# First group of a delta-rule attention: 16x16 lane inverses joined on TensorE, and its later pieces moved among its steps

## The reference, cut to what matters

```python
k_n = k / (np.linalg.norm(k, axis=-1, keepdims=True) + 1e-06)
for t in range(S):
    kt, vt, bt = (k_n[:, :, t], v[:, :, t], beta[:, :, t, None])
    y[:, :, t] = np.einsum('bhd,bhde->bhe', q[:, :, t], state)
    v_old = np.einsum('bhde,bhd->bhe', state, kt)
    state = state + bt[:, :, :, None] * np.einsum('bhd,bhe->bhde', kt, vt - v_old)
```

## Time and profile before

| | |
|---|---|
| median of 3 runs | 909.62 us (909.47 to 911.56) |
| profiled execution, its own time | 913.28 us |
| its span | 911.5 us |
| PE busy (92%) | 837.3 us |
| DVE busy | 477.4 us |
| ACT busy | 301.5 us |
| POOL busy | 199.2 us |
| DMA queue q1, 32802 packets | 63.85 MB |
| DMA queue q8, kind "instruction", 69 packets | 1.13 MB |

### The profile page before, as it was taken

How to read it: one execution, slowest core, us unless ns; L and a number is a source line. 1 busy time by engine, 2 the same in 40 slices (tenths; PEclk the granted TensorE clock), 3 DMA queues, 4 the chain that set the end, 5 groups by cost and what they waited for, 6 DMA issues and landing times.

```text
span 911.5 us, 24639 instructions
## 1 busy us (share of the span) xinstructions
PE 837.3 (92%) x10634; PEld 811.5 (89%) x10634; DVE 477.4 (52%) x1092; ACT 301.5 (33%) x654; POOL 199.2 (22%) x167
## 2 busy tenths in 40 slices
PE   6378889899986799999999999999999999999998
PEld 6268888898885799999999999999889999899898
DVE  5999987979465574424442543433542432432421
ACT  4147374656532212211111211123441331331422
POOL 3123122031200530800270010000132222132231
PEclk9657787987978799999999999999999999999999
DMA  9600506134145121022000201201510010000001
GB/s 362 164 37 23 202 30 196 37 106 140 64 160 165 53 63 59 18 70 69 17 9 9 69 17 49 78 16 64 194 53 27 26 52 26 26 0 26 27 1 53
DMA packets 32889, 65.13 MB, mean 71 GB/s; under 512 B 3673, under 2 KB 25506, under 8 KB 32802
## 3 DMA queue, kind: packets, MB, share of 16 engines
q1 hardware_dynamic: 32802, 63.85, 20.8%
HBM read 46.86 MB, written 14.16 MB: 67 GB/s over the span
## 4 chain that ended last, share of the span: by engine, by line
PE 60%; issue 21%; DVE 11%; ACT 4%; POOL 2%; DMA 1%; SPq 1%; POOLq 0%; ACTq 0%; DVEq 0%
PE m_ps_h L1090 12%; PE g_ps_v L1601 11%; PE m_ps_d L1090 10%; PE ps_ga L404 4%; PE g_ps_y L1601 3%; PE ps_y L495 3%; PE ps_y L490 3%; DVE t_lane L584 2%; DVE prod L580 2%; PE ps_u L473 2%; PE ps_r L455 2%; POOL g_vn_lo L1498 2%; PE g_ps_u L1601 2%; PE ps_s L508 2%; ACT tt L327 2%
## 5 line engine op out<-in xcount | busy, mean ns | idle before, releaser
L1090 PE MATMUL m_ps_h<-m_unt_hi,m_w_hi 128*128 128x256 f32 x432 | 122.3, 283 | 2.8 <-DVE m_unt_lo L1280 2.1
L1090 PE MATMUL m_ps_h<-m_unt_lo,m_w_hi 128*128 128x256 f32 x432 | 121.4, 281 | 0.0
L1090 PE MATMUL m_ps_h<-m_unt_hi,m_w_lo 128*128 128x256 f32 x432 | 121.4, 281 | 0.0
L1286 DVE SCALAR_TENSOR_TENSOR m_h_lo<-m_ps_h,m_h_hi 128x512 fp32r<-128x512 f32 x72 | 49.8, 692 | 107.0 <-ACT m_h_hi L990 107.0
L1090 PE MATMUL m_ps_d<-m_w_hi,m_h_hi 128*128 128x384 f32 x288 | 97.6, 339 | 0.0
L1090 PE MATMUL m_ps_d<-m_w_hi,m_h_lo 128*128 128x384 f32 x288 | 96.4, 335 | 0.0
L1090 PE MATMUL m_ps_d<-m_w_lo,m_h_hi 128*128 128x384 f32 x288 | 96.3, 334 | 0.0
L990 ACT ACTIVATE m_h_hi<-m_ps_h 128x512 fp32r<-128x512 f32 x72 | 43.1, 598 | 150.8 <-PE m_ps_h L1090 150.8
L1090 PEld LDWEIGHTS m_ps_h<-m_unt_hi,m_w_hi 128*128 128x128 f32 x432 | 82.0, 190 | 3.4 <-DVE m_unt_lo L1280 2.5
L1090 PEld LDWEIGHTS m_ps_h<-m_unt_hi,m_w_lo 128*128 128x128 f32 x432 | 83.1, 192 | 0.0
L1090 PEld LDWEIGHTS m_ps_h<-m_unt_lo,m_w_hi 128*128 128x128 f32 x432 | 82.1, 190 | 0.0
(11 more groups left out here) (220 smaller groups left out, 1947.6 us busy)
## 6 DMA issues: line engine op xcount, KB each, us to landing
kq<-kq_g SPq DMA_DIRECT2D x24, 512.0 KB, 7.0
v_in<-v_g SPq DMA_DIRECT2D x6, 768.0 KB, 8.7
k_in<-k_g SPq DMA_DIRECT2D x6, 768.0 KB, 10.6
x_scr<-y_sb SPq DMA_DIRECT2D x24, 192.0 KB, 1.9
stage<-w_ch SPq DMA_DIRECT2D x6, 768.0 KB, 8.7
x_scr<-m_x_sb SPq DMA_DIRECT2D x24, 192.0 KB, 1.9
g_x<-x_scr SPq DMA_DIRECT2D x24, 192.0 KB, 4.4
out<-g_y SPq DMA_DIRECT2D x24, 192.0 KB, 1.9
```

What stands on the lines that cost most here:

```text
L1090: last = pe.matmul(out, first[x], second[y], start=(k == 0 and m == 0), stop=(k == n - 1 and m == 2))
L1286: dve.scalar_tensor_tensor(h_lo[:, 2 * g:2 * g + 2].rearrange("p f t -> p (f t)"), ps_h[g % 2][:, :], 0.0, h_hi[:, 2 * g:2 * g + 2].rearra ...
```

## The change

Group 0 alone is inverted another way. PE first multiplies the 128 diagonal 32x32 blocks of the keys straight into the bank pair `ps_y` (`first_diagonals`); DVE transposes from there, without the three copies. In the lanes only the two 16x16 blocks on the diagonal of each are scaled and inverted, 15 columns of both at once. PE then joins them to the 32x32 inverse: `fine_preset` puts the unit matrix into a bank, `fine_blocks` does "v", "c" and "r", 64 matmuls of 32x32 for each half, with ACT copying each result out. ACT's table for the root is loaded at the start by a root of one element. FIRST ends with "g" 1; the pieces "a" 1 and "g" 2, the couplings w(0, 1) and x(0, 1) and half of the corners stand among the steps of group 0. `to_lanes(1)` stands behind `unlanes(0)`. POOL scales v of group 0 after the last column. `below` and `v_fine` are other names for `w_sb` and for half of `score[1]`.

```diff
-    FIRST = (("g", 0), ("a", 0), ("g", 1), ("a", 1), ("g", 2))
+    FIRST = (("g", 0), ("a", 0), ("g", 1))
     uses = [(what, g, p) for what, g in FIRST for p in range(4)]
-    uses += [("w", 0, 0), ("w", 0, 1), ("x", 0, 0), ("x", 0, 1)]
+    uses += [("v", 0, 0), ("v", 0, 1), ("c", 0, 0), ("r", 0, 0), ("w", 0, 0), ("x", 0, 0), ("c", 0, 1), ("r", 0, 1)]
...
+        if i == 0 and n < 4:
+            uses += [("g", 2, n)]
+        if 2 <= n < 6 and i + 1 < G:
...
-        if i and n == 1:
+        if n == 1:
...
-        if i and n == 2:
+        if n == 2:
...
+        diag_done, below_zero, below_ok = sem("diag_done"), sem("below_zero"), sem("below_ok")
+        unit_ok, rows_ok, one_ok = sem("unit_ok"), sem("rows_ok"), sem("one_ok")
...
+        below, v_fine = w_sb, score[1][:, 0:HU].rearrange("p a (b s) -> p (a b) s", s=H)
...
+            return FINE_LINKS + (g - 1) * LINKS if g else 0
...
-                pool.wait_ge(chain, g * LINKS + 2 * AHEAD + 4)
+                pool.wait_ge(chain, links(g) + 2 * AHEAD + 4 if g else links(1))
...
+            pool.memset(below[:], 0.0).then_inc(below_zero, 1)
+            pool.wait_ge(below_zero, 1)
+            for a in range(4):
+                pool.tensor_copy(unit[quarter(a)], ident[quarter(a), H * a:H * a + H]).then_inc(unit_ok, 1)
+            pool.wait_ge(unit_ok, 4)
             for p in range(2):
                 pool.memset(tt[p][:], 0.0).then_inc(tt_zero, 1)
             pool.wait_ge(tt_zero, 2)
-            pool.wait_ge(ident_ok, 2)
-            pool.wait_ge(ga_out, turn["g", 0, 3] + 1)
-            pool.tensor_copy(g_diag[quarter(3)], gram_sb[0][quarter(3), 1]).then_inc(dg_pool, 1)
-            pool.wait_ge(dg_pool, 1)
...
-                pool.wait_ge(chain, (g + 1) * LINKS)
+                pool.wait_ge(chain, links(g + 1))
...
+            def fine(what, out, c, after):
+                m = turn[what, 0, c]
+                act.wait_ge(ga_done, turn[after, 0, c] + 1)
+                act.activation(out[:, HU * c:HU * c + HU], coupling(m, slice(0, P)), ACT.Copy).then_inc(ga_out, 1)
+
+            def first_corners(c):
+
+                us = slice(HU * c, HU * c + HU)
+                act.wait_ge(ga_out, turn["c", 0, c] + 1)
+                act.wait_ge(tt_zero, 2)
+                for a in range(4):
+                    last = act.activation(tt[0][quarter(a), us, H * (a % 2):H * (a % 2) + H], t_cols[quarter(a), us],
+                                          ACT.Copy)
+                last.then_inc(corner_ok, 1)
+
+            act.wait_ge(one_ok, 1)
+            act.activation(one[:, 1:2], one[:, 0:1], ACT.Sqrt)
             for p in range(4):
                 piece("g", 0, p)
-            act.wait_ge(ga_out, 4)
-            act.activation(g_diag[quarter(1)], gram_sb[0][quarter(1), 1], ACT.Copy).then_inc(dg_act, 1)
+            roots(0)
+            act.wait_ge(glane_ok, 1)
+            act.wait_ge(below_zero, 1)
+            act.wait_ge(rows_ok, 5)
+            act.activation(below[:, :, Q:H], ps_y[:, :].rearrange("p (u t) -> p u t", t=H)[:, :, Q:H], ACT.Identity,
+                           scale=upper_rows[:]).then_inc(below_ok, 1)
             for what, g in FIRST[1:]:
                 for p in range(4):
                     piece(what, g, p)
-                    if (what, g, p) == ("a", 0, 1):
-                        roots(0)
+            fine("v", v_fine, 0, "v")
+            fine("v", v_fine, 1, "v")
             roots(1)
+            fine("c", t_cols, 0, "r")
+            fine("r", t_rows, 0, "r")
             solved_w(0, 0)
-            solved_w(0, 1)
-            corners(0, 0)
+            first_corners(0)
             solved_x(0, 0)
-            solved_x(0, 1)
-            corners(0, 1)
+            fine("c", t_cols, 1, "r")
+            fine("r", t_rows, 1, "r")
...
-                if i and 2 <= n < 6 and i + 1 < G:
+                if i == 0 and n < 4:
+                    piece("g", 2, n)
+                if 2 <= n < 6 and i + 1 < G:
...
-                if 0 < i < G - 1 and n == 1:
+                if i < G - 1 and n == 1:
                     solved_w(i, 1)
-                if 0 < i < G - 1 and n == 2:
+                if i == 0 and n == 1:
+                    first_corners(1)
+                if i < G - 1 and n == 2:
                     solved_x(i, 1)
...
-                pe.wait_ge(trows_ok, g + 1)
+                if g:
+                    pe.wait_ge(trows_ok, g + 1)
+                else:
+                    pe.wait_ge(ga_out, turn["r", 0, c] + 1)
...
-                pe.wait_ge(tcols_ok, g + 1)
+                if g:
+                    pe.wait_ge(tcols_ok, g + 1)
+                else:
+                    pe.wait_ge(ga_out, turn["c", 0, c] + 1)
...
+            def first_diagonals():
+
+                for c in range(2):
+                    pe.wait_ge(kq_in[0][0][c], 16)
+                    for u in range(HU * c, HU * c + HU):
+                        for a in range(4):
+                            x = kq[0][C * (a // 2):C * (a // 2) + C, 0, u, H * (a % 2):H * (a % 2) + H]
+                            last = pe.matmul(ps_y[quarter(a), H * u:H * u + H], x, x, start=True, stop=True)
+                last.then_inc(diag_done, 1)
+
+            def fine_preset(c):
+                m = turn["v", 0, c]
+                bank_free(m)
+                pe.matmul(ps_ga[m % 2][:, 0:HU * H], ident[:], unit[:].unsqueeze(1).broadcast_to([P, HU, H]),
+                          start=True, stop=False, skip_group_check=True)
+
+            def fine_blocks(what, c, left, right, **how):
+
+                m = turn[what, 0, c]
+                for j in range(HU):
+                    for a in range(4):
+                        u = HU * c + j
+                        last = pe.matmul(coupling(m, quarter(a))[:, j], left[quarter(a), u], right[quarter(a), u], stop=True,
+                                         **how)
+                last.then_inc(ga_done, 1)
+
+            def fine_half(c):
+
+                bank_free(turn["c", 0, c])
+                pe.wait_ge(ga_out, turn["v", 0, c] + 1)
+                fine_blocks("c", c, v_fine, t_cols, start=True)
+                bank_free(turn["r", 0, c])
+                fine_blocks("r", c, t_cols, v_fine, start=True)
+
+            first_diagonals()
             for what, g in FIRST:
                 for p in range(4):
                     piece(what, g, p)
+            pe.wait_ge(ident_ok, 2)
+            pe.wait_ge(unit_ok, 4)
+            fine_preset(0)
+            fine_preset(1)
+            pe.wait_ge(below_ok, 1)
+            pe.wait_ge(trows_ok, 1)
+            for c in range(2):
+                fine_blocks("v", c, below, t_rows, start=False, skip_group_check=True)
+            pe.wait_ge(tcols_ok, 1)
+            fine_half(0)
             couple_w(0, 0)
-            couple_w(0, 1)
             couple_x(0, 0)
-            couple_x(0, 1)
-            pe.wait_ge(ident_ok, 2)
+            fine_half(1)
...
-                        pe.wait_ge(corner_ok, 2 * (g + 1))
+                        pe.wait_ge(corner_ok, 2 * (g + 1) if g else c + 1)
...
-                if i and 2 <= n < 6 and i + 1 < G:
+                if i == 0 and n < 4:
+                    piece("g", 2, n)
+                if 2 <= n < 6 and i + 1 < G:
...
-                if i and n == 1:
+                if n == 1:
                     couple_w(i, 1)
-                if i and n == 2:
+                if n == 2:
                     couple_x(i, 1)
...
-                    dve.wait_ge(dg_dve, 2)
-                    dve.wait_ge(dg_act, 1)
-                    dve.wait_ge(dg_pool, 1)
-                dve.transpose(g_lane[g % 2][:], g_diag[:].rearrange("p u s -> p s u")).then_inc(glane_ok, 1)
+                    dve.wait_ge(diag_done, 1)
+                source = g_diag[:] if g else ps_y[:, :].rearrange("p (u s) -> p u s", s=H)
+                dve.transpose(square(g_lane[g % 2]), source.rearrange("p u s -> p s u")).then_inc(glane_ok, 1)
...
+                dve.tensor_copy(t_lane[:, 0:H * H:H + 1], scale[:]).then_inc(chain, 1)
+                if g:
+                    blocks = ((square(g_lane[g % 2]), scale[:].unsqueeze(2).broadcast_to([P, H, H])),)
+                else:
+                    blocks = [(square(g_lane[0])[:, at:at + Q, at:at + Q],
+                               scale[:, at:at + Q].unsqueeze(2).broadcast_to([P, Q, Q])) for at in (0, Q)]
+                for block, rows in blocks:
+                    last = dve.scalar_tensor_tensor(block, block, -1.0, rows, ALU.mult, ALU.mult)
+                last.then_inc(chain, 1)
+                dve.wait_ge(chain, links(g) + 2)
...
+            def fine_column(j):
+
+                m, n = Q - 1 - j, j + 1
+                x = prod[:, 0:2 * m * n].rearrange("p (b i k) -> p b i k", b=2, k=n)
+                g, t = diagonal_pair(g_lane[0]), diagonal_pair(t_lane)
+                rest = t[:, :, j + 1:Q, 0:n]
```

(57 more changed lines are left out.)

13 lines of the change are left out of this document (3 added, 10 removed).

## The result

| | before | after |
|---|---|---|
| median | 910.03 us (909.47 to 911.56, 4 runs) | 923.70 us (921.60 to 925.37, 4 runs) |
| profiled execution, its own time | 913.28 us | 922.81 us |
| its span | 911.5 us | 920.7 us |
| start of the first u | 58.09 us | 62.88 us |
| start of w(1, 0) | 81.27 us | 90.89 us |

The change makes the kernel slower: ratio 1.0146, 95% interval 1.012 to 1.0173. DVE has 18 us less work, and the kernel takes 13.7 us more by the medians, 9.2 us more by the two profiled spans. The median of 923.70 us lies inside the forecast range by 0.3 us (its upper end is 924.0), and above the 914.5 to 922.5 of the main case.

A forecast was written before the change was run, and what follows sets the result against it. PE was taken as the bound, its instructions arriving in blocks of 128 records at 3.9 us. w(1, 0) moves from 81.27 to 90.8, 9.5 later, less 0.2: 909.62 + 9.3 = 918.9 us, range 912.5 to 924.0.

The forecast's parts named there:

- main case: Whole kernel: added instruction blocks of 3.5 to 4.1 us each slow it to 914.5 to 922.5 us; chance 0.72.
- 514 matmuls more are eight blocks: PE up to w(1, 0): 1028 added records arrive in blocks of 128, at 3.9 us each 31 us of supply.
- 6.9 blocks, 26.9 us: Steps of group 0, record 1572 to w(1, 0): 882 records at the supply's pace, reaching 90.3 us.
- Rival 1: Instruction supply is hidden, only engines count: first u at 47.3, w(1, 0) at 76.4, time 903.5 us; chance 0.10.
- rival 2: No change: hidden supply, but fine blocks at 28 ns a record, 3.6 us each; first u 55.4, time 911; chance 0.07.
- The end that I had at 28.6: Start of the kernel: block 608 was to take 5.6 us, between 3.9 and 8.39, and end at 28.6 us.
- Rival 4: DVE's columns of both blocks cost as before: `t_rows` at 40, 3 us more, 922 us; chance 0.03.
- rival 3: Slower still: early blocks take 8.39 us behind full DMA, first matmuls at half clock, ACT needs another table; chance 0.08.
- I take 9.3: Whole kernel: w(1, 0) moves 9.5 us later, 0.2 is lost in one stall; on the median 918.9 us.
- steps and stalls repeat: Behind w(1, 0): DVE has 8 us of slack before w(2, 0), and only 0.2 us of the shift is lost.
- Both paths reach w(1, 0) together: Seam to group 1: PE's steps end at 90.8 and DVE, waiting for group 2's diagonals, has `t_rows(1)` at 90.4.
- I priced the diagonals on PE through the root alone: Start of group 0: diagonals in front of the pieces cost 3.7 us, ACT's root ending at 19.0 against 15.33.

The follow-up runs named there:

- the version with pairs: Against the kernel after: no first_diagonals, "g" 2 early, "r" transposed on DVE, "v" as 64 matmuls of 64x64; 906.66 us, ratio 0.9966 to the kernel before.

## Why the prediction was right, and where it was not

**Supply, right up to the first u.** The step that carried the sum was that 514 matmuls more are eight blocks and that blocks, not columns, set the time after "v". In the fine stage, up to the first u, that is shown. The packets (77), the windows of 128 records, the run with a quarter of the columns and the one with twice the instructions all say so. Behind the first u it is not what happened: I had 6.9 blocks, 26.9 us, there, and the stretch took 28.0 us with PE busy 26.24 of them and only 0.37 us of "issue". That a record of work costs about as much there (32 ns) as a block's share (3.9 us for 128, 30 ns) made the figure fit; that part of the agreement is luck. Rival 1 (hidden supply) and rival 2 (28 ns a record; 216 fine records took 2.04 us, 9.4 ns each) are out. In the fine stage five of the six ends of blocks show an idle of 1.35 to 3.85 us; the sixth (52.40, 0.29 us) stands behind two waits for ACT. So the crossing of a block is not hidden in the fine stage, and nearly is in the steps behind it (0.37 us in 28.01). On four tiles side by side the 216 records above are 18.9 ns for each matmul of two records, at a granted clock of 1.00.

**Step by step.** Block ends 11.61, 17.74 and 23.82 (I had 11.2, 17.0 and 23.0), root of group 0 ends 19.7 (I had 19.0), first column 22.6 (22.2), `t_rows` ready 33.3 (32.9), block ends 39.35, 43.07, 46.53, 52.40, 56.12 and 59.58 (39.3, 43.2, 47.1, 52.5, 56.4, 60.3), first u 62.9 (63.4), last "g" 2 piece copied 75.6 (75.5), diagonals at DVE 82.0 (81.9), `t_rows` of group 1 ready 89.8 (90.4), w(1, 0) 90.9 (90.8). The profiled execution took 922.81 us, where I had 922.6. The end that I had at 28.6 shows no idle. Inside that, sizes were off and cancelled: a block at idle DMA engines took 3.46 to 3.73 us there, not 3.9; the one with the waits for the copies of "r" and w took 5.87, where I had 5.4, and the steps 28.0, where I had 27.4. Rival 4 did not happen: the columns ran from 22.62 to 31.24. Nor did rival 3, which I had at 925 us and whose start the upper end of the range took in: the longest early block took 6.1 us (17.74 to 23.82), not 8.39, and the granted clock, 0.50 from 39.34 to 59.58, was 1.00 from 65.40 to 90.89, so already ahead of iteration 3; ACT loaded one table only, at 0.81 us.

**The size, too small.** The step that failed is the last term of the sum, "I take 9.3 ... on the median: 909.62 + 9.3". The medians differ by 13.7 us, and 9.3 lies below the interval of the ratio (10.9 to 15.7 us). Two things are behind it. First, "steps and stalls repeat" holds only on average: w(2, 0) came 12.3 us later than before (w(1, 0) 9.6) and w(5, 0) 12.6, and the last group then gave 3 back, while the second execution ended only 7.2 us later (spans 918.1 and 910.9). Second, the profiled executions of before (913.28, 912.83) lie near the top of their kernel's times, and that of after (922.81, among 921.60 to 925.37) does not. I took off 3.66 us for the first and had no reason to expect the same of the second. Which of the two carries more stays open; the second execution of the kernel after (920.28) lies 10.4 us above the median of the kernel before beside it (909.91).

**Wrong in its reasoning.** "Both paths reach w(1, 0) together, so mending one alone gives nothing": putting "g" 2 back took three pieces out of the stretch behind the first u as well, and gave 3.0 us at w(1, 0), all on the path over PE; on the one over DVE `t_rows` came 15 us earlier and gave nothing by itself. And I priced the diagonals on PE through the root alone, which the run without them supports (3.3 us at "v"), while I expected two whole blocks of that run. The two views must not be mixed: before a wait for another engine only lateness at the wait counts (with two blocks fewer PE stood 6.31 us for `t_rows` instead of 1.18), behind it every record that PE does not get in time (3.9 us a block in the run with twice the instructions).

## What to carry to other kernels

Count PE's instructions as well as its columns: here 64 small fp32 matmuls (128 records with their loads) took 3.45 to 4.3 us in the fine stage, though PE was busy 1.9 us of it, and 6.5 beside a bulk load. Where 128 records keep PE busy longer than that, as in the steps (32 ns a record), the supply cost next to nothing (0.37 of 28.01 us). Work taken from an engine for which PE waits and given to PE as many small tiles may shorten the wait and lengthen the stream behind it; merge tiles (the version with pairs, 3.8 us by the medians), let another engine transpose instead of multiplying a second time, and keep bulk loads out of stretches of small matmuls (6.47 us a block beside one, 3.72 without). Where PE is about to stand for another engine, instructions in front of the wait are free: with two blocks fewer PE stood 6.31 us there instead of 1.18.
